# Storing each whole tile of the outcome by one transfer over all 128 rows in place of four over 32

## What is computed

```python
# q, k, v: (2, 12, 448, 64); w_in: (768, 2048); w_out: (2048, 768), two of each
scores = cap * np.tanh(scale * np.matmul(q, k.transpose(0, 1, 3, 2)) / cap)
attn = np.exp(scores - np.max(scores, axis=-1, keepdims=True))
attn = attn / (np.sum(attn, axis=-1, keepdims=True) + 1e-09)
x = np.matmul(attn, v)                 # then (B, H, S, D) -> (B * S, H * D)
x = np.maximum(x @ w_in1, 0.0) ** 2 @ w_out1
h = x @ w_in2
return h * (1.0 / (1.0 + np.exp(-h))) @ w_out2
```

## Time and profile before

| what | us |
|---|---|
| median of 3 runs | 532.4 |
| lowest, highest | 532.11, 532.63 |
| the profiled execution, its own time | 531.69 |
| its span, first to last instruction | 529.9 |
| TensorE busy in the span | 521.0 |
| VectorE busy | 350.9 |
| ScalarE busy | 260.3 |
| GpSimd busy | 77.5 |

### The profile page before, as it was taken

How to read it: one execution, slowest core, us unless ns; L and a number is a source line. 1 busy time by engine, 2 the same in 40 slices (tenths; PEclk the granted TensorE clock), 3 DMA queues, 4 the chain that set the end, 5 groups by cost and what they waited for, 6 DMA issues and landing times.

```text
span 529.9 us, 7052 instructions
## 1 busy us (share of the span) xinstructions
PE 521.0 (98%) x2628; PEld 440.0 (83%) x2628; DVE 350.9 (66%) x604; ACT 260.3 (49%) x404; POOL 77.5 (15%) x52
## 2 busy tenths in 40 slices
PE   7999999999999999999999999999999999999996
PEld 5333335799999999999999999999999999999996
DVE  3487878797687533667799746556764245568975
ACT  5999996154454333544444344454444144454220
POOL 1899999000000000000000000000000000000000
PEclk9999999999999999999999999999999999999999
DMA  7798611051302202522032025202211241020447
GB/s 222 196 241 227 180 41 33 28 141 59 80 0 80 59 1 59 141 59 67 13 80 61 1 61 139 61 18 62 60 49 32 61 138 36 26 80 10 102 74 106
DMA packets 82181, 42.17 MB, mean 80 GB/s; under 512 B 26848, under 2 KB 79072, under 8 KB 82144
## 3 DMA queue, kind: packets, MB, share of 16 engines
q1 hardware_dynamic: 77984, 40.32, 29.2%
q10 hardware_dynamic: 4128, 1.38, 1.1%
q0 software_dynamic: 32, 0.00, 0.0%
HBM read 38.93 MB, written 2.75 MB: 79 GB/s over the span
## 4 chain that ended last, share of the span: by engine, by line
PE 94%; DMA 2%; DVE 1%; ACT 1%; issue 1%; SPq 1%; ACTq 0%
PE banks L558 27%; PE banks L557 27%; PE banks L559 27%; PE banks L477 4%; PE banks L470 4%; PE banks L498 2%; PE banks L467 1%; DMA qk_raw<-in_k_dram 1%; DMA qk_raw<-in_q_dram 1%; PE banks L489 1%; ACT prob L683 1%; SPq L324 1%; ACT prob L690 0%; DVE asum L917 0%; ACTq L660 0%
## 5 line engine op out<-in xcount | busy, mean ns | idle before, releaser
L557 PE MATMUL banks<-x_hi,w_hl 128*128 128x448 f32 x384 | 139.4, 363 | 0.0
L558 PE MATMUL banks<-x_lo,w_hl 128*128 128x448 f32 x384 | 139.4, 363 | 0.0
L559 PE MATMUL banks<-x_hi,w_hl 128*128 128x448 f32 x384 | 138.3, 360 | 0.0
L558 PE MATMUL banks<-g_lo,w_hl 128*128 128x448 f32 (+1 forms) x340 | 122.7, 361 | 0.0
L557 PE MATMUL banks<-g_hi,w_hl 128*128 128x448 f32 (+1 forms) x340 | 122.5, 360 | 0.0
L559 PE MATMUL banks<-g_hi,w_hl 128*128 128x448 f32 (+1 forms) x340 | 121.7, 358 | 0.0
L557 PEld LDWEIGHTS banks<-x_hi,w_hl 128*128 128x128 f32 x384 | 72.1, 188 | 6.9 <-issue 1.4
L559 PEld LDWEIGHTS banks<-x_hi,w_hl 128*128 128x128 f32 x384 | 71.8, 187 | 5.1
L558 PEld LDWEIGHTS banks<-x_lo,w_hl 128*128 128x128 f32 x384 | 72.1, 188 | 3.8
L975 DVE TENSOR_TENSOR w_hl<-w_raw,w_hl 128x768 fp32r<-128x768 f32 x32 | 31.9, 996 | 55.4 <-ACT w_hl L716 55.2
L557 PEld LDWEIGHTS banks<-g_hi,w_hl 128*128 128x128 f32 x340 | 63.8, 188 | 4.8
(11 more groups left out here) (63 smaller groups left out, 509.8 us busy)
## 6 DMA issues: line engine op xcount, KB each, us to landing
w_raw<-in_moe_w_in_dram SPq DMA_DIRECT2D x32, 384.0 KB, 3.4
w_raw<-in_moe_w_out_dram SPq DMA_DIRECT2D x24, 512.0 KB, 5.2
qk_raw<-in_k_dram SPq DMA_DIRECT2D x44, 112.0 KB, 2.7
qk_raw<-in_q_dram SPq DMA_DIRECT2D x44, 112.0 KB, 3.3
v_t<-in_v_dram SPq DMA_DIRECT2D x24, 96.0 KB, 2.8
out_dram<-rows SPq DMA_DIRECT2D x38, 56.0 KB, 2.2
qk_raw<-in_k_dram ACTq DMA_DIRECT2D x4, 112.0 KB, 3.0
qk_raw<-in_q_dram ACTq DMA_DIRECT2D x4, 112.0 KB, 4.0
```

The costliest lines, as they stand in the source:

```text
L557: pe.matmul(dst, hi[:, kk, :], mov_hi, start=start, stop=False, skip_group_check=onto)
L558: pe.matmul(dst, hi[:, kk, :], mov_lo, start=False, stop=False, skip_group_check=onto)
L559: return pe.matmul(dst, lo[:, kk, :], mov_hi, start=False, stop=stop, skip_group_check=onto)
```

## The change

A whole tile is stored by one transfer instead of four. `out_tiles[m, b]` is the outcome seen as column block a, row (i t), feature r, and the on-chip side is all of `rows[m][:, b, :]`. SP issues the eight tiles of groups 0 and 1 that way. In the last group SP takes tiles n = 0 and 2 whole and ScalarE takes n = 1 whole. The two parts of the last tile are stored as before, two transfers from either engine for each part. The count at the end is that of 11 whole tiles and 8 partial transfers. Nothing else differs; no instruction of TensorE, VectorE or GpSimd is touched.

```diff
     out_v = out.rearrange("(b i t) m -> b i t m", b=B, t=QB)
+    out_by_tile = out.rearrange("(b x) (m a r) -> b m a x r", b=B, r=BL, a=C)
+    out_tiles = {(m, b): out_by_tile[b, m].rearrange("a (i t) r -> a i t r", t=QB) for m in range(KC) for b in range(B)}
...
+        def part_out(m, b, a, t):
+            return out_v[b, :, t, m * P + BL * a:m * P + BL * a + BL]
+
+        def part_rows(m, b, a, t):
+            return rows[m][BL * a:BL * a + BL, b, :].rearrange("p (t r) -> p t r", r=BL)[:, t, :]
...
-            def store(m, b, a, t=slice(0, QB)):
-                cols = slice(m * P + BL * a, m * P + BL * a + BL)
-                sp.dma_start(out_v[b, :, t, cols],
-                             rows[m][BL * a:BL * a + BL, b, :].rearrange("p (t r) -> p t r", r=BL)[:, t, :]
-                             ).then_inc(s_out, DMA)
-
             for g in range(GROUPS):
-                for n in range(3 if g == GROUPS - 1 else 4):
+                for n in range(4):
+                    if g == GROUPS - 1 and n in (1, 3):
+                        continue
+                    sp.wait_ge(s_rows, 4 * g + n + 1)
                     m, b = y_tile(g, n)
-                    sp.wait_ge(s_rows, 4 * g + n + 1)
-                    for a in range(2 if g == GROUPS - 1 else C):
-                        store(m, b, a)
+                    sp.dma_start(out_tiles[m, b], rows[m][:, b, :]).then_inc(s_out, DMA)
+            m, b = y_tile(GROUPS - 1, 3)
             for part, t in enumerate(LAST_T):
                 sp.wait_ge(s_rows, 4 * GROUPS + part)
                 for a in range(2):
-                    store(*y_tile(GROUPS - 1, 3), a, t)
-            sp.wait_ge(s_out, DMA * (B * KC * C + C))
+                    sp.dma_start(part_out(m, b, a, t), part_rows(m, b, a, t)).then_inc(s_out, DMA)
+            sp.wait_ge(s_out, DMA * (B * KC - 1 + 2 * C))
...
-            for n in range(3):
-                act.wait_ge(s_rows, 4 * (GROUPS - 1) + n + 1)
-                for a in range(2, C):
-                    store(*y_tile(GROUPS - 1, n), a)
+            act.wait_ge(s_rows, 4 * (GROUPS - 1) + 2)
+            m, b = y_tile(GROUPS - 1, 1)
+            act.dma_start(out_tiles[m, b], rows[m][:, b, :]).then_inc(s_out, DMA)
+            m, b = y_tile(GROUPS - 1, 3)
             for part, t in enumerate(LAST_T):
                 act.wait_ge(s_rows, 4 * GROUPS + part)
                 for a in range(2, C):
-                    store(*y_tile(GROUPS - 1, 3), a, t)
+                    act.dma_start(part_out(m, b, a, t), part_rows(m, b, a, t)).then_inc(s_out, DMA)
```

## The result

The changed kernel takes 562.03 us (median of 6 runs, 561.82 to 563.45) against 532.3 for the kernel before in the same session: a ratio of 1.0559, 95% interval 1.0549 to 1.0570, 29.7 us slower. The forecast was 573.0, with a range of 560 to 600; time and range agree, the point was 11 us too high. The profiled execution has a span of 560.4 us.

A forecast was written before the change was run, and what follows sets the result against it. TensorE's matmuls bound the kernel, busy 521.0 of 529.9 us. Stores on four engines, from 498.5 for 71.1 us, end at 569.6; the span becomes 570.5, 40.6 longer, so 532.4 + 40.6 = 573.0 us, range 560 to 600.

The forecast's parts named there:

- Nothing moves before the last transpose, and no store is in anyone's way: Up to 526.45 us the kernel runs as before; no load queues behind a store, only SP's last wait needs stores landed.
- Four engines, from an outermost count of 4: Whole-tile stores, memory side 4x448x32: cutting only the outermost loop gives four DMA engines 448 pieces each; chance 0.79 at 564 to 600.
- Never dry, 5040 pieces on each of four engines: Store queue from 498.5 us: tiles become ready faster than four engines store them, at 6.3 us a tile, so no gaps.
- The price of a piece, 14.1 ns: DMA engine time per 128-byte store piece, the middle of 13.6 and 14.6 ns; 5040 pieces make 71.1 us.
- My lower bound: Store pieces may overlap on an engine as weight loads do, share 1.15: 12.3 ns a piece, 62.0 us, total 563.9.
- the signs for four engines: Expected in the changed profile from 498.5 to about 569 us: DMA share 0.25 to 0.27, rate 35 to 37 GB/s.
- The 0.55 us to be had from fewer issues: At the end, SP's last two stores could start at 526.5 and 527.0 instead of from 527.07: at most 0.55 us gained.
- Point (1) of the prediction: Fewer store issues, each costed at 0.6 us: SP saves 17 us, nearly all beside TensorE's work; at most 0.55 us gained.
- The rival with sixteen engines: Whole-tile stores still spread over 16 engines: 531.9 to 532.4 us, no difference; chance 0.14, of which 0.02 faster by over 0.2%.
- point (4) of the prediction: SP and ScalarE queues feed the same engines: only order changes, a held-up SP delays nothing else, and the 0.55 us gain goes.
- SP's last wait of 43 us and landing times over 40 us: Expected at the end: SP's closing wait some 43 us, issue-to-landing time growing from 7 us to over 40 for the last tile.
- One engine at a time: Rival: a transfer's shares are written out in turn and hardly overlap, 25.3 us a tile, 781 in all; partly so shares 0.07.

## Why the prediction was right, and where its size was off

- **Nothing moves before the last transpose, and no store is in anyone's way:** right. Busy times agree within 0.4 us, and the whole loss lies behind 527.0.
- **Four engines, from an outermost count of 4:** right, and the deciding step. It was a choice between two ends; no row of before showed it. The packets show 4 completions a tile, and the counts 16, 8, 4, 2 give as many engines. The Trainium skill ("DMA: Bandwidth & Descriptors", "Why a DMA increments its semaphore by 16 and not by 1") states this rule, and here the runs agree with it, for the counts 16, 8, 4 and 2 of the memory side; nothing between these counts was tried. Its advice in "Rules for kernel authors", one transfer over 128 partitions in place of two over halves, because both halves go over all 16 engines, does not carry over to quarters here. The quarter transfers do go over all sixteen, but the whole tile does not: 532.3 us against 562.03. Two halves of this pattern go over two engines each, and are slower still, 619.37 us.
- **Never dry, 5040 pieces on each of four engines:** right; from 500 to 558 the rate is 46 GB/s on the mean, and no slice of 1.6 us in it is below 37.
- **The price of a piece, 14.1 ns:** this term was mis-sized. 5040 pieces went from 499.0 to about 559.5, 12.0 ns each on the average, 60.5 us instead of 71.1; those 10.6 us are nearly all of the 11 us by which the point was too high. My lower bound, 12.3 ns from the overlap that the weight loads show, was nearly it, and I chose the nearer rows instead: same pieces, but sixteen engines. The flaw was to read a busy share divided by pieces as a price. The engines overlap pieces, so the share says how long pieces are open, not how many an engine could take. That the price was equal in thin and full stretches looked like proof that it belonged to the engine; with four engines a piece is open longer (0.38 x 16 x 20 us / 7031 pieces = 17.3 ns) and yet they follow each other on an engine every 11.4 ns. The same mistake gave the signs for four engines, a share of 0.25 to 0.27 and 35 to 37 GB/s, where 0.36 to 0.39 and 43 to 45 were measured.
- **The 0.55 us to be had from fewer issues:** this gain did not come. That the stores of the tile before keep SP busy is borne out: the last issue comes 1.12 us behind the rows, and the end follows it by 2.3 us. But with sixteen engines and a third of the issues the time is the same (1.0000), and there an issue is held for 1.33 us. Point (1) of the prediction had reckoned every issue at 0.6 us, whatever stands before it in the queue. The rival with sixteen engines was priced at 531.9 to 532.4, no difference, and its run gave that. In the changed kernel the term does not count, as point (4) of the prediction said.
- **SP's last wait of 43 us and landing times over 40 us:** not seen. SP was held in its issues instead, 5.3 us in the middle, and the profile gives no landing time for these transfers. For the sum it made no difference, as point (4) of the prediction had it for the case that the queue fills.
- **One engine at a time:** did not happen; two, four and eight engines work side by side, and the rate grows as their number (22, 45, 89 GB/s).

## What to carry to other kernels

Before several transfers are merged, look at the outermost loop of the memory side's pattern after folding: with counts from 2 to 16 it set here how many DMA engines carry the transfer, and the 128 rows of on-chip memory on the other side did not help. Fewer issues gained nothing here as long as every piece was stored. Count the completion packets of a queue to see how many engines a transfer had. And a busy share is no price: take the rate of a stretch with a backlog, with the same number of engines at work. And before a late end is put down to one engine, find the last issue of every engine that issues.

## What was not expected of the hardware

- An engine takes a piece of 128 bytes every 11.4 to 12.0 ns, whether two, four or eight are at work (22, 45, 89 GB/s). Sixteen reach 139 to 164 GB/s, 12.5 to 14.7 ns. What holds sixteen back was not tried.
- The issue of a transfer is not always 0.6 us: behind a backlog it lasts in the middle as long as the engines take for one transfer's share, 5.3 us with four engines (448 pieces), 10.5 us with two (896) and 5.2 us with two and half tiles (448), and everything behind it on SP waits.

```profile
L417 SPq DMA_DIRECT2D out_dram<-rows x10: 685/10488/19639, 500.3 to 595.5; - x10
```

That row is of the run with outermost count 2. With count 16 the same issue takes 610 ns in the middle:

```profile
L417 SPq DMA_DIRECT2D out_dram<-rows x10: 557/610/2100, 497.6 to 524.6; - x10
```
